# Regrouping the recurrence stages of a fused kernel: nine shared bank groups, work of three chunks in one period

## The reference, cut to what matters

```python
# 1. recurrence, per batch and head, state is 40 x 40
for t in range(S):
    y[:, :, t] = einsum('bhd,bhde->bhe', rt, state)
    Sa = einsum('bhde,bhe->bhd', state, at)
    state = state * wt[:, :, None, :] - einsum('bhd,bhe->bhde', Sa, bt) + einsum('bhd,bhe->bhde', vt, kt)
# 2. mixing over time (rank 32) and over channels (320 -> 1280 -> 320)
u = x + (x.T @ U @ V).T
x = u + max(u @ w_ch1, 0) @ w_ch2
# 3. four causal attention "experts", two chosen per token by a gate
for e in range(E): out += mask_e * w_e * (softmax(q_e @ k_e.T / 8) @ v_e @ wo_e)
```

## Time and profile before

| | us |
|---|---|
| median of 3 runs (1312.17 to 1313.52) | 1312.38 |
| the profiled execution | 1306.82 |
| its span | 1305.0 |
| recurrence alone, to the first `z` | 213 |
| three stretches of recurrence and mixing, ended by the next `z` | 320, 311, 290 |
| mixing of the last batch alone | 171 |

### The profile page before, as it was taken

The page is one execution under the profiler, slowest core; times in us unless marked ns, Lnnn a source line. Parts: engine busy times, 40 slices in busy tenths (PEclk is TensorE's granted clock), DMA queues, the critical chain, the costliest instruction groups (busy, mean ns, idle before and its releaser), DMA issues.

```text
span 1305.0 us, 55200 instructions
## 1 busy us (share of the span) xinstructions
PE 1130.3 (87%) x24816; PEld 841.8 (65%) x24816; DVE 568.0 (44%) x1209; ACT 393.2 (30%) x1014; POOL 297.2 (23%) x543
## 2 busy tenths in 40 slices
PE   4877778999997888999899888899999887899977
PEld 4766667666575667766567666766667666555555
DVE  4454544333235664343234575533224575310265
ACT  1333333322122433322122354332122354210044
POOL 3444443222222221222222122222122122000000
PEclk9888898999997886999899798899999899999989
DMA  8222322111111111111111111211111110000000
GB/s 267 69 80 77 90 81 72 51 42 53 36 55 45 43 60 47 59 43 52 54 38 48 49 48 58 65 44 55 40 38 56 35 50 28 27 0 1 1 12 21
DMA packets 47625, 68.25 MB, mean 52 GB/s; under 512 B 19616, under 2 KB 34528, under 8 KB 47392
## 3 DMA queue, kind: packets, MB, share of 16 engines
q1 hardware_dynamic: 47392, 64.72, 16.7%
HBM read 56.83 MB, written 7.86 MB: 50 GB/s over the span
## 4 chain that ended last, share of the span: by engine, by line
PE 75%; DVE 9%; issue 8%; ACT 6%; DMA 0%; POOL 0%; DVEq 0%; ACTq 0%; SPq 0%; POOLq 0%
PE PB L981 12%; PE PB L769 11%; PE PB L1000 8%; PE PB L776 6%; PE PB L1017 5%; PE PB L1044 4%; PE PB L1060 3%; ACT R L434 2%; PE PB L758 2%; PE PB L1010 2%; PE PB L1036 2%; PE PB L1069 2%; PE PB L989 2%; ACT work L519 2%; PE PB L729 1%
## 5 line engine op out<-in xcount | busy, mean ns | idle before, releaser
L387 POOL TENSOR_TENSOR QI<-R,consts 128x256 f32<-128x256 f32 x192 | 146.3, 762 | 315.5 <-ACT R L434 219.7
L434 ACT COPY R<-PB 128x672 f32<-128x672 f32 x192 | 98.3, 512 | 303.1 <-PE PB L776 234.8
L769 PE MATMUL PB<-R 64*64 64x64 f32 x5376 | 135.8, 239 | 43.2 <-ACT R L434 23.3
L769 PEld LDWEIGHTS PB<-R 64*64 64x64 f32 x5376 | 110.3, 147 | 86.3 <-issue 67.4
L981 PE MATMUL PB<-uf,W 128*128 128x384 f32 x480 | 160.3, 488 | 4.7 <-ACT uf L485 4.7
L981 PEld LDWEIGHTS PB<-uf,W 128*128 128x128 f32 x480 | 89.0, 190 | 62.0 <-issue 5.5
L1000 PE MATMUL PB<-work,W 128*128 128x384 f32 x320 | 108.0, 495 | 0.0
L439 ACT COPY R<-PB 128x384 f32<-128x384 f32 x96 | 46.0, 479 | 156.8 <-PE PB L776 156.8
L414 POOL TENSOR_TENSOR BK<-EA,INV 128x160 f32<-128x160 f32 x96 | 49.0, 531 | 182.3 <-DVE INV L586 182.3
L418 POOL TENSOR_TENSOR M<-UP,consts 128x128 f32<-128x128 f32 x48 | 21.9, 456 | 288.1 <-DVE UP L594 288.1
L1044 PE MATMUL PB<-consts,work 128*128 128x128 f32 x336 | 68.0, 332 | 22.5 <-DVE work L669 13.3
(11 more groups left out here) (130 smaller groups left out, 2058.4 us busy)
## 6 DMA issues: line engine op xcount, KB each, us to landing
EA<-ea_dram SPq DMA_DIRECT2D x48, 498.0 KB, 3.6
LA<-la_dram SPq DMA_DIRECT2D x48, 384.0 KB, 3.4
VT<-vt_dram SPq DMA_DIRECT2D x48, 80.0 KB, 1.8
x_mid_dram<-XO SPq DMA_DIRECT2D x192, 20.0 KB, 1.9
xs<-x_mid_dram SPq DMA_DIRECT2D x24, 160.0 KB, 2.8
out_dram<-ob SPq DMA_DIRECT2D x24, 160.0 KB, 1.8
W<-w_dram SPq DMA_DIRECT2D x1, 1600.0 KB, 13.3
W<-w_dram SPq DMA_DIRECT2D x1, 1280.0 KB, 9.0
```

What stands on the lines that cost most here:

```text
L387: nc.gpsimd.tensor_tensor(QI[j][:].rearrange("p (u g t) -> p u g t", u=2, g=2), src, eye3.unsqueeze(1).to_broadcast([P, 2, 2, C]), ALU.add ...
L434: freed(nc.scalar.copy(dst[:].rearrange("p (u c) -> p u c", u=2), pair(what, n)[:, :, 0:cols]), 1, what, n)
L769: mm = nc.tensor.matmul(out[half(m1), u, lo:lo + C], left, right, start=True, stop=True)
```

## The change

The 16 stages become nine groups that share a bank pair each, and the pairs of stages in a group belong to different chunks. A period now works on `r1` to `r3` of chunk i, `r4` to `r6` of chunk i-1, `r7`, `U`, `X`, `ST`, `o1` of chunk i-2 and `o2`, `o3` of chunk i-3 (before: chunks i and i-1), with keys prepared one and decays two chunks ahead. The groups stand in three clusters (A, B, C), and a stage that needs another's result stands one cluster or more behind it. Mixing has fixed places, `mix`, between the clusters; attending steps may stand behind a group or a `mix`. With mixing, the recurrence has always two bank pairs, layer 2 and the projections have four banks, attending steps two.

```diff
-PERIOD = (("r3", 0), ("U", 0), ("o2", -1), ("r4", 0), ("s2", 1), ("scan", 2),
-          ("r5", 0), ("o3", -1), ("s3", 1), ("r6", 0), ("s1", 2), ("den", 2),
-          ("r7", 0), ("r1", 1), ("X", 0), ("r2", 1), ("ST", 0), ("o1", 0), ("inv", 2), ("bk", 2))
-TURNING = ("s1", "s2", "o1")
+BK_DEPTH, PT_DEPTH, END_DEPTH, AF_DEPTH, XV_DEPTH, VK_DEPTH, OB_DEPTH = 5, 5, 5, 4, 4, 3, 3
+LEAD = {"scan": 2, "bk": 1, "den": 2, "inv": 2,
+        "r1": 0, "r2": 0, "r3": 0, "r4": -1, "r5": -1, "r6": -1, "r7": -2,
+        "U": -2, "X": -2, "ST": -2, "o1": -2, "o2": -3, "o3": -3, "s1": 2, "s2": 1, "s3": 1}
+MEMBERS = {"A1": ("r4", "r7"), "A2": ("r1",), "A3": ("U", "o2"),
+           "B1": ("r2", "r5"), "B2": ("X", "o3"), "B3": ("s2", "s1"),
+           "C1": ("r3", "r6"), "C2": ("s3", "ST"), "C3": ("o1",)}
+PERIOD = ("bk", "A1", "A2", "A3", "scan", "mix", "B1", "B2", "B3", "mix", "den", "C1", "C2", "inv", "C3", "mix")
...
-    starts = [own.index(("o1", NC * (b + 1))) for b in range(B - 1)]
+    starts = [own.index(("A1", NC * (b + 1) + 3)) for b in range(B - 1)]
...
-            if mixing[k][0] in ATTENDING or step[0] in TURNING:
+            if step[0] == "mix" or mixing[k][0] in ATTENDING and step[0] in MEMBERS:
...
-            slots = (0, 1, 2, 3) if j < ALONE else (0, 1) if attending else (0, 1, 2)
+            slots = (0, 1, 2, 3) if j < ALONE else (0, 1)
...
-            slots = (10, 11, 6, 7) if last else (10, 11)
+            slots = (10, 11, 6, 7) if last else (10, 11) if attending else (8, 9, 10, 11)
```

```diff
+            def second(group, i, tile):
+                is_full(act, group, i)
+                freed(nc.scalar.copy(tile[:, 8 * C:16 * C], PB[PLACE[group, i][0]][:, 1, :]), group, i)
+            def first(group, i, tile):
+                is_full(dve, group, i)
+                freed(nc.vector.tensor_copy(tile[:, 0:8 * C], PB[PLACE[group, i][0]][:, 0, :]), group, i)
+            def spread(n):
+                act.wait_ge(inv_made, n + 1)
+                if n >= 1:
+                    act.wait_ge(bk_made, n)
+                for p in range(2):
+                    for j in range(2):
+                        nc.scalar.copy(INB[half(p ^ j), p * TOK:(p + 1) * TOK], INV[half(p), :]).then_inc(inv_spread, 1)
+            def turn_m1(n):
+                taken(dve, "s3", n)
+                for p in range(2):
+                    lo = 4 * C + p * 2 * C
+                    nc.vector.tensor_tensor(gt(M1[1][half(1 - p), :]), gt(UP[half(p), lo:lo + 2 * C]),
+                                            eye.unsqueeze(1)[half(p)].to_broadcast([C, 2, C]), ALU.add
+                                            ).then_inc(m1_turned, 1)
+            def taken(eng, what, n):
+                is_out(eng, GROUP[what], n - LEAD[what])
```

The keys b and k, which stood in two tiles of columns, now stand one on each half of the 128 rows, and so do X and V (`XV`, loaded with V, X copied into it). Matmuls over 64 rows that added two results, or gave two results of the same operand, become one over 128 rows or with 128 columns:

```diff
-                for g, p, u in HEADS:
-                    lo = 4 * C + (2 * g + u) * C
-                    nc.tensor.matmul(out[feat(u), p, g * D:g * D + D], at(BK, n)[half(p), lo:lo + D],
-                                     at(VT, n)[half(p), packed(g, u)], start=(g == 0), stop=False, skip_group_check=True)
-                is_out(pe, "X", n)
-                for g, p, u in HEADS:
-                    mm = nc.tensor.matmul(out[feat(u), p, g * D:g * D + D], at(BK, n)[half(p), spaced(g, u)],
-                                          XS[half(p), spaced(g, u)], start=False, stop=True, skip_group_check=True)
+            def update(n, out):
+                taken(pe, "X", n)
+                for g, p, u in HEADS:
+                    mm = nc.tensor.matmul(out[feat(u), p, 6 * C + g * D:6 * C + g * D + D], at(BK, n)[:, head_of(p, g, u)],
+                                          at(XV, n)[:, head_of(p, g, u)], start=True, stop=True)
```

More of the change, by code:

```diff
@@ L45, with chunk_of, drains_of @@
 LATE = 8000
+def chunk_of(what, i):
+    n = i + LEAD[what]
+    return n if 0 <= n < N else None
 def recurrent_steps():
     steps = []
[L51 to L56, removed]
-    return steps
+    for i in range(-2, N + 3):
+        for what in PERIOD:
+            if what == "mix" or any(chunk_of(x, i) is not None for x in MEMBERS.get(what, (what,))):
+                steps.append((what, i))
+            if what == "B2" and (i + LEAD["o3"]) % 2 == 1 and chunk_of("o3", i) is not None:
+                n = chunk_of("o3", i)
+                steps.append(("xs", n // NC, n % NC // 2))
+    return steps
+def drains_of(what, *args):
+    if what in MEMBERS:
+        i, = args
+        ops = {"U": 1, "o2": 1, "X": 2, "o3": 1, "s2": 1, "s1": 2, "s3": 2, "ST": 1, "o1": 2}
+        if what in ("A1", "A2", "B1", "C1"):
+            return 2
+        return sum(ops[x] for x in MEMBERS[what] if chunk_of(x, i) is not None)
+    if what == "score" or what in ("u", "x2") and args[1] == 2:
+        return 2
+    return 1
 def mixing_steps(b):
@@ L127, in places @@
         what = step[0]
-        last = what not in IN_PAIRS and step[1] == B - 1
+        last = what not in MEMBERS and step[1] == B - 1
         if what in ATTENDING or what in IN_BANKS:
             attending = what in ATTENDING
-        if what in IN_PAIRS:
-            slots = (0, 1, 2, 3) if j < ALONE else (0, 1) if attending else (0, 1, 2)
+        if what in MEMBERS:
+            slots = (0, 1, 2, 3) if j < ALONE else (0, 1)
         elif what == "score":
@@ L152, in places @@
             users[i] = step
-        at[step] = slot, uses[slot], banks
         uses[slot] += 1
+        out_of[slot] += drains_of(*step)
+        at[step] = slot, uses[slot], banks, out_of[slot]
     return at, before
@@ L250, in feat, with partly_out, freed, sent @@
             return slice(C * j, C * j + D)
-        def pair(what, n):
-            return PB[PLACE[what, n][0]]
         def is_full(eng, *step):
-            slot, use, banks = PLACE[step]
-            eng.wait_ge(full[slot], use + 1)
+            slot, use, banks, target = PLACE[step]
+            eng.wait_ge(full[slot], use)
         def is_out(eng, *step):
[L260 to L267, removed]
+            slot, use, banks, target = PLACE[step]
+            eng.wait_ge(drained[slot], target)
+        def partly_out(eng, ops, *step):
+            slot, use, banks, target = PLACE[step]
+            eng.wait_ge(drained[slot], target - drains_of(*step) + ops)
+        def freed(op, *step):
+            op.then_inc(drained[PLACE[step][0]], 1)
+        def taken(eng, what, n):
+            is_out(eng, GROUP[what], n - LEAD[what])
+        def sent(eng, b):
+            if b > 0:
+                for j in range(OB_DEPTH):
+                    eng.wait_ge(written[j], 16 * NT * b // OB_DEPTH)
         def gt(ap):
@@ L323, in _ @@
             load_ea(1)
-            for n in range(3):
-                load_vt(n)
+            for n in range(XV_DEPTH):
+                load_xv(n)
             for n in range(2):
@@ L769, in square, with extend @@
-                        mm = nc.tensor.matmul(out[half(m1), u, lo:lo + C], left, right, start=True, stop=True)
-                return mm
-            def extend(j, out, lo, Qi, Qi_per, M, M_per, M_lo):
+                        col = to + (2 * x + g) * C
+                        mm = nc.tensor.matmul(out[half(m1), u, col:col + C], left, right, start=True, stop=True)
+                return mm
+            def extend(j, out, to, M, lo):
+                per = M.shape[1] // 2
                 for g, p, u in HEADS:
@@ new lines, in round2, with round3 @@
+            def round2(n, out):
+                taken(pe, "r1", n)
+                return square(2, out, 0, R1, 0)
+            def round3(n, out):
+                taken(pe, "r2", n)
+                square(3, out, 0, R25, 0)
+                pe.wait_ge(m1_made, n + 1)
+                pe.wait_ge(m1_turned, 2 * n + 2)
+                pe.wait_ge(qi_made[1], n + 1)
+                for g, p, u in HEADS:
+                    lo = g * C + (1 - u) * p * 2 * C
+                    mm = nc.tensor.matmul(out[half(p), u, 4 * C + g * C:4 * C + g * C + C],
+                                          QI[1][half(p ^ u), u * 2 * C + g * C:u * 2 * C + g * C + C],
+                                          M1[u][half(p ^ u), lo:lo + C], start=True, stop=True)
+                return mm
```

799 lines of the change are left out of this document (417 added, 382 removed).

## The result

The changed kernel takes 1367.6 us (1361.4 to 1368.7, 4 runs) against 1312.3 (1302.1 to 1313.5): a ratio of 1.043, 95% interval 1.038 to 1.048. It is slower. The forecast was 1236 with a range to 1316. Its profiled execution has a span of 1359.6 us (before 1305.0).

| us | alone, to first z | stretch 1 | stretch 2 | stretch 3 | last batch alone |
|---|---|---|---|---|---|
| before | 213 | 319 | 311 | 290 | 171 |
| after | 251 | 319 | 319 | 299 | 172 |
| forecast | 219 | three stretches together 83 less | | | 171 |

What follows compares the result with a forecast made beforehand. Half of each 14.6 us period was taken as not array work: instruction fetches and short groups waiting for drains. 1306.8 + 6 - 14 - 35 - 34 + 1 = 1231, timed 1236 us, range 1168 to 1316.

Steps and rivals of the forecast that it cites:

- TensorE's work: Array time of a chunk: 7.4 us against 7.3, no array time saved; 6.6 to 9.2 with the bounds.
- Fetches and shapes: Per chunk: 14% fewer fetches save 0.4 us, in the recurrence alone at most; added shape changes cost 0.3.
- The recurrence alone: Before the first `z`: a period of 13.8 us against 14.6, first `z` at 219 us instead of 213.4 (+6).
- clock term: In a period of the recurrence alone: the clock adds 0.6 us to the chain.
- first four periods 32.5 us: Start of the recurrence alone: four partial periods take 5.5 + 7 + 9 + 11 us, ahead of 13 at 13.8.
- The stretches with layer 2: 22 chunks beside layer 2 and projections: 9.0 us each, saving 1.6 as `mix` covers the chain: -35 us.
- Attention: 14 chunks in the attending stretches: 9.0 us each, from 11.4: -34 us (0 to -60).
- The slower one: Rival: VectorE-to-ScalarE chain in series makes a period alone 17.1 us, first `z` +49, timed 1365; chance 0.14.
- thin cover: In the stretches, part of the 0.14 rival: where cover is thin, 0.5 us a chunk is lost, +18.
- The 128-row records in turns: Rival: 128-row loads and matmuls alternate, 0.105 us a record, 2.5 us a chunk, +90, timed 1326; chance 0.04.

## Why the prediction was wrong

**TensorE's work (the step that failed first).** I put 64 wide records at 0.027 us, one price for four forms, and forgot that X and V would lie on two quarters. Measured by the starts of the weight loads at full clock: 40 rows x 128 columns 0.054, 128 x 64 0.027, 128 x 40 0.018, and X and V 0.027 to 0.031 instead of 0.015 to 0.016. So the price was right for one form, too high for one and half of the truth for the 32 records of `s3` and `o2`. Instead of 7.4 against 7.3 us, the array part of a chunk is 9.3 against 7.9. The bounds that I gave (6.6 to 9.2) end just below it, and the sum did not use them: 1.4 us in the 34 to 36 chunks beside mixing are 50 us, more than the whole saving from gaps. The narrow matmuls show 1.1 of it. The rest wasn't undone; by the forms' distances it is X and V (+0.5) and two transposes (+0.2), less what `r7` gained on four quarters (-0.2). That X and V would slow down could have been read from `r7` in the trace before.

**Fetches and shapes.** 174 fetches against 175 forecast, 21840 records as forecast. The stalls fell by more than the 0.4 us a chunk that I had at most, from 29 to 10 us in the twelve periods alone, but behind the wait for ScalarE that gained nothing. The added shape changes are in the array part and weren't measured apart.

**The recurrence alone.** The chain was the right one, in the right order. A period at full clock takes 13.6 to 13.9 us, where the sum without its clock term has 13.2 (the two `M1` instructions of VectorE take 1.03 us together, and I had put in 0.6). So the 13.8 is hit in part by luck. The mean is 15.1: five periods with 3 to 12 us at 1.2 GHz take 16.5 to 17.5, while four with some 5 us of it take 13.3 to 13.9. All that is 1.3 us a period above those at full clock, and I had +0.6, as if the clock would stay at 0.87. It fell to 0.83. The term "first four periods 32.5 us" was too small as well: the first `SN` comes at 62.7, where 7 + 32.5 and the greater part of a period give some 52. Together +32 us on the 219. `spread` behind A3 takes 30 us away, so this loss was one of order, not of the cut into groups.

**The stretches with layer 2.** Gaps fell by 1.0 us a chunk, where the sum had taken 2.0 off (of 3.3 it kept 0.5 and 0.8, shapes aside): right in kind, half as large. The two pairs of banks cost 0.4 of it, of which I had written that the wait inside a cluster is all they cost.

**Attention.** The -34 us had no mechanism of its own: I took the chunk's cost from the other stretches. The gaps there did not fall (31 to 36 us a window against 26 to 31). The larger part, 23 of 31.7 us in the first window, ends on `exp` and the copies of attention itself (L582, L569). That two works' times add up, as (352-192)/14 showed, does not tell that the recurrence's waits are the ones that cost; the waits by line hinted at it before (L1036 and L1044 on L519, 11.5 of 31 us in the first window). Neither freer places nor half of `exp` shortened the windows beyond the noise, so why this term failed stays open.

**The rivals.** The slower one named the place (INV, `spread`, A1's copy, R1) and came out at 1365, but its reason for the stretches, thin cover, is not what happened: there it was array time. That its total is so near is luck, since its period was 17.1 us and the measured one 15.1. The 128-row records in turns would have been 0.105 us apart; they are 0.018 and 0.027, so that rival is out. (The rule behind it, in the Trainium skill, "TensorE: Matmul & The Clock Gate", Part 3, is that weight loads run beside matmuls only for other rows; the trace does not agree with it here.) What did cost in `s3` and `o2` was the number of columns of the weights: 0.054 us at 128 columns, 0.027 at 64 and 0.018 at 40, with 64, 40 and 40 moving ones. The same page of the Trainium skill (Part 2, on LDWEIGHTS) says that a load's time goes with its columns and not with its rows, and the trace agrees: the 128 columns lie on 40 rows, the 64 and 40 on all 128. (Where the moving columns are more, as in L1060, they set the distance; see the last section.)

## What to carry to other kernels

Halving the number of small matmuls by making each twice as wide saves no array time where weights are used once: here 16 records of 128 columns took 1.0 us and 32 of 64 took 0.57. It can save fetches, and these counted only where nothing else filled TensorE (11 us in the recurrence alone, once ScalarE no longer held it up), so by these numbers the two parts want different forms, which no run tried. Price each form by the distance of starts of its nearest row with the same number of stationary and moving columns and the same quarters of the array, and write the sum at both ends before choosing. In a list that all engines follow in order, look for an instruction that waits for another engine's last work of a period (here `spread` for INV) ahead of drains that are ready. A wait of 2 us in every period was worth its own length, 1.9 us a period; the higher clock that came with its removal showed up as some 2 us in all.

## What the runs showed of the hardware that was not expected

Matmuls of 64 x 64 on two of the four quarters of the array are 0.027 to 0.031 us apart whether neighbours share a quarter or alternate (on four quarters 0.014 to 0.016). Weight load and matmul over 40 rows and 128 columns with 64 moving columns take 0.054 us, as much as an L1060 record of 128 rows, 64 columns and 128 moving columns; with 64 columns and 40 moving ones (L990) it is 0.027. So in these three forms the distance went with the larger of the two numbers, and L1060 was a fit row for 128 columns though it has 64.

Each pause of TensorE at "issue" of over 0.5 us in the twelve periods alone (25 in the kernel before, 9 in the changed one) ended 1.1 to 1.6 us after a packet of instructions had landed.
